# Router's logits in four groups of token tiles, behind the output projection of token tile 0

## What is computed

```python
def phi(x):                                   # 8 heads, 64 wide, 128 features
    proj = einsum('bhsd,df->bhsf', x, w_phi)
    proj = proj - max(abs(proj), axis=-1)
    return concatenate([exp(proj), exp(-proj)])
num, den = phi(q) @ (phi(k).T @ v), phi(q) @ sum(phi(k))
x = num / (den + 1e-6)                        # linear attention, then 512 wide

gate = sigmoid(causal 5-tap convolution of x, per channel)
x = (gate * (x @ w_val)) @ w_out              # gated block

logits = x @ w_gate                           # 8 experts, top 1
local  = sigmoid(x @ w_local)                 # >= 0.5: keep the expert of the token before
out[s] = softmax(logits[s])[e] * (relu(x[s] @ w1[e]) @ w2[e])
```

## Time and profile before

| | us |
|---|---|
| median of 3 runs (lowest to highest) | 531.75 (531.22 to 534.05) |
| the profiled execution | 531.9 |
| its span | 530.2 |

### The profile page before, as it was taken

The page is one execution under the profiler, slowest core; times in us unless marked ns, Lnnn a source line. Parts: engine busy times, 40 slices in busy tenths (PEclk is TensorE's granted clock), DMA queues, the critical chain, the costliest instruction groups (busy, mean ns, idle before and its releaser), DMA issues. The chain is left out here.

```text
span 530.2 us, 13320 instructions
## 1 busy us (share of the span) xinstructions
PE 510.3 (96%) x5374; PEld 431.7 (81%) x5374; DVE 301.5 (57%) x492; ACT 261.8 (49%) x450; POOL 220.5 (42%) x224
## 2 busy tenths in 40 slices
PE   6999999999999999999999999999999999999993
PEld 5898999988989999678887787888887777888872
DVE  4686878878986554287505657422375578522231
ACT  2555676666786331564625556322555557422330
POOL 3069999999999950436620001100111011100001
PEclk9999999999999999999999999999999999999998
DMA  8466464654510000006669399111382977111101
GB/s 298 133 201 208 139 227 157 203 189 139 165 70 1 0 1 1 1 1 205 253 239 337 106 351 339 61 40 40 102 295 50 348 278 265 41 40 42 53 25 43
DMA packets 31351, 75.34 MB, mean 142 GB/s; under 512 B 4159, under 2 KB 4415, under 8 KB 31296
## 3 DMA queue, kind: packets, MB, share of 16 engines
q1 hardware_dynamic: 25600, 60.37, 33.8%
q0 software_dynamic: 3104, 9.46, 4.6%
q10 hardware_dynamic: 2592, 4.74, 3.1%
HBM read 57.46 MB, written 17.55 MB: 141 GB/s over the span
## 5 line engine op out<-in xcount | busy, mean ns | idle before, releaser
L568 POOL TENSOR_TENSOR gate<-gate,tap 128x576 f32<-128x576 f32 x64 | 93.1, 1455 | 5.3
L612 POOL DMA_INDIRECT out_rows<-o_sb,meta_cur x18 | 18.6, 1033 | 151.5 <-DVE o_sb L1448 151.5
L1435 DVE TENSOR_TENSOR h_t<-pair_ps,h_t 128x512 fp32r<-128x512 f32 x36 | 24.9, 691 | 88.5 <-ACT h_t L1175 88.5
L662 PE MATMUL turn<-wts,h_t 128*128 128x512 f32 x144 | 60.0, 417 | 1.4 <-issue 1.4
L662 PE MATMUL num_ps<-wts,y_t 128*128 128x512 f32 x144 | 59.5, 413 | 0.1
L663 PE MATMUL turn<-wts,h_t 128*128 128x512 f32 x144 | 56.9, 395 | 0.0
L663 PE MATMUL num_ps<-wts,y_t 128*128 128x512 f32 x144 | 56.9, 395 | 0.0
L664 PE MATMUL turn<-wts,h_t 128*128 128x512 f32 x144 | 56.9, 395 | 0.0
L664 PE MATMUL num_ps<-wts,y_t 128*128 128x512 f32 x144 | 56.9, 395 | 0.0
L1209 DVE TENSOR_REDUCE absmax<-pair_ps 128x8 f32<-128x1024 f32 x31 | 38.0, 1225 | 29.8 <-PE pair_ps L671 29.8
L1167 ACT ACTIVATE h_sb<-num_ps 128x512 f32<-128x512 f32 x36 | 21.5, 598 | 65.6 <-PE num_ps L664 65.6
(11 more groups left out here) (210 smaller groups left out, 1117.6 us busy)
## 6 DMA issues: line engine op xcount, KB each, us to landing
ring<-in_w SPq DMA_DIRECT2D x36, 512.0 KB, 6.9
stage<-in_w SPq DMA_DIRECT2D x28, 512.0 KB
kq_t<-in_kq SPq DMA_DIRECT2D x15, 576.0 KB, 6.4
sorted_rows<-padrow SPq DMA_DIRECT2D x9, 771.0 KB, 5.7
v_sb<-in_v_aug SPq DMA_DIRECT2D x16, 325.0 KB, 3.2
ysl<-sorted_rows ACTq DMA_DIRECT2D x18, 257.0 KB
wout_t<-in_w_out_t SPq DMA_DIRECT2D x1, 1024.0 KB, 7.9
wval_sb<-in_w_val SPq DMA_DIRECT2D x1, 1024.0 KB, 9.5
```

The lines of the kernel that those rows point to most:

```text
L568: nc.gpsimd.tensor_tensor(g, g, tap[:, t % 2, :], ALU.add).then_inc(conv_step, 1)
L662: nc.tensor.matmul(dst, x[0], w[0], start=first, stop=False)
```

## The change

The constants: four groups of token tiles instead of three, the first two of 5 tiles and the others of 4. So the first piece is 4 groups of 512 columns, the second 2 groups of 128. The logits are computed behind tile 0 of the output projection instead of before it, and are transposed behind the second channel group of tile 1 instead of behind tile 0: five transposes, of 128 rows (the last of 64) instead of six of 96. The routing steps begin one tile later. ScalarE rounds tiles 0 and 1 as soon as the first batch is gated (in its queue that is behind the work of the last batch), into the buffers that do not overlap the weights of the value projection: `rounded(t)` turns the four buffers by two. The copy of the transposed logits becomes five instructions. GpSimd takes the low parts of 11 tiles instead of 9 and does its `iota` behind the fourth of them, no longer behind the last value tile. VectorE takes 7, the early weight chunks move by two tiles, and the eighth is subtracted behind the last low part.

```diff
-    LG = 3
-    LGS = TOK // LG
-    LGT = TT // LG
+    LG = P // LGW
+    LG_TILES = [TT // LG + (j < TT % LG) for j in range(LG)]
+    LG_AT = [sum(LG_TILES[:j]) for j in range(LG)]
+    LGT = LG_TILES[0]
+    LGS = LGT * P
+    WIDE = TT % LG
+    LG_HALF = 3
...
-        lg_pieces = [(kv_ps, slice(0, 512)), (num_ps[:, 0, :], slice(512, LGS))]
+        lg_pieces = [(kv_ps, slice(0, 512), LG), (num_ps[:, 0, :], slice(512, LGS), WIDE)]
...
-        POOL_LO = TT // 2
+        POOL_LO = TT // 2 + 2
         early_at = [i if i < STAGES else POOL_LO + 2 + i - STAGES for i in range(EARLY)]
...
+        EARLY_OUT = 2
+        def rounded(t):
+            return gs[(t + GS - EARLY_OUT) % GS]
...
-            pool.wait_ge(val_ok, B * 2 * CT)
-            nc.gpsimd.iota(ytok[:, :, C:C + 1].bitcast(I32), pattern=[[P, TT], [0, 1]], base=0,
-                           channel_multiplier=1).then_inc(conv_step, 1)
-            pool.wait_ge(conv_step, done + 1)
             for t in range(POOL_LO):
                 pool.wait_ge(g_hi, t + 1)
                 whole, (hi, lo) = split_gated(t)
                 nc.gpsimd.tensor_tensor(lo, whole, hi.bitcast(F32), ALU.subtract).then_inc(g_lo[0], 1)
+                if t == GS - 1:
+                    nc.gpsimd.iota(ytok[:, :, C:C + 1].bitcast(I32), pattern=[[P, TT], [0, 1]], base=0,
+                                   channel_multiplier=1).then_inc(conv_step, 1)
+            pool.wait_ge(conv_step, done + 1)
...
-            pe.wait_ge(gated_ok, B * 2 * CT)
-            for bank, at in lg_pieces:
-                w = at.stop - at.start
-                for c in range(CT):
-                    for j in range(LG):
-                        ins = nc.tensor.matmul(bank[j * LGW:(j + 1) * LGW, 0:w], wog[:, c, :],
-                                               gate[:, c, j * LGS + at.start:j * LGS + at.stop],
-                                               start=(c == 0), stop=(c == CT - 1))
-                ins.then_inc(lg_ok, 1)
+            def logits():
+                pe.wait_ge(gated_ok, B * 2 * CT)
+                for bank, at, groups in lg_pieces:
+                    w = at.stop - at.start
+                    for c in range(CT):
+                        for j in range(groups):
+                            ins = nc.tensor.matmul(bank[j * LGW:(j + 1) * LGW, 0:w], wog[:, c, :],
+                                                   gate[:, c, LG_AT[j] * P + at.start:LG_AT[j] * P + at.stop],
+                                                   start=(c == 0), stop=(c == CT - 1))
+                    ins.then_inc(lg_ok, 1)
...
                     if c == CT - 1:
                         ins.then_inc(y_ok, 1)
-                    if c % 2 == 1 and 0 <= 2 * t + c // 2 - 4 < len(routing):
-                        route(*routing[2 * t + c // 2 - 4])
+                    if t == 1 and c == 1:
+                        turn_logits()
+                    if c % 2 == 1 and 0 <= 2 * t + c // 2 - 6 < len(routing):
+                        route(*routing[2 * t + c // 2 - 6])
                 if t == 0:
-                    turn_logits()
+                    logits()
...
+            act.wait_ge(gated_ok, 2 * CT)
+            for t in range(EARLY_OUT):
+                round_gated(t)
             act.wait_ge(gated_ok, B * 2 * CT)
-            for t in range(GS):
+            for t in range(EARLY_OUT, GS):
                 round_gated(t)
-            for i, (bank, at) in enumerate(lg_pieces):
-                act.wait_ge(lg_ok, i + 1)
-                nc.scalar.copy(lg_rows[:, at], bank[0:LG * LGW, 0:at.stop - at.start]).then_inc(lg_read, 1)
             for t in range(TT):
                 act.wait_ge(y_ok, t + 1)
                 nc.scalar.copy(ytok[:, t, 0:C], turn_ps[t % 2][:]).then_inc(y_read, 1)
                 if t == 0:
+                    for i, (bank, at, groups) in enumerate(lg_pieces):
+                        act.wait_ge(lg_ok, i + 1)
+                        nc.scalar.copy(lg_rows[0:groups * LGW, at], bank[0:groups * LGW, 0:at.stop - at.start]).then_inc(lg_read, 1)
                     act.wait_ge(lg_ok, len(lg_pieces) + 1)
...
+                    read_logits()
...
                 if t - POOL_LO < EARLY:
                     rest_of_weights(t - POOL_LO)
+            for i in range(TT - POOL_LO, EARLY):
+                rest_of_weights(i)
```

More of the change, by code:

```diff
@@ L81, in attention_moe_kernel @@
     FEWT = E * FEW // P
-    LGT = TT // LG
-    assert LG * LGT == TT and LGT % 2 == 0 and E + 1 <= LGW
+    LG = P // LGW
[5 more added lines that the diff above has]
+    LG_HALF = 3
+    assert 0 < WIDE and LG_HALF < LGT - 1 and 512 < LGS < 1024 and (LGT - 1) * P == 512 and E + 1 <= LGW
     assert PAIRS == B * CT and FEAT == P and FULL * P + HALF == S and FULL * P == 512
@@ L398, in split_gated @@
         def split_gated(t):
-            return gate[:, :, t * P:(t + 1) * P], [gs[t % GS][:, i] for i in range(2)]
+            return gate[:, :, t * P:(t + 1) * P], [rounded(t)[:, i] for i in range(2)]
+        EARLY_OUT = 2
+        def rounded(t):
+            return gs[(t + GS - EARLY_OUT) % GS]
         block = ctx.enter_context(nc.Block())
@@ L820, in turn_logits @@
                 for i in range(LGT):
-                    ins = nc.tensor.transpose(lgt_ps[i // (LGT // 2)][:, i % (LGT // 2) * LG * LGW:(i % (LGT // 2) + 1) * LG * LGW],
-                                              lg_rows[:, i * P:(i + 1) * P], ident[0:LG * LGW, 0:LG * LGW])
+                    rows = P if i + 1 < LGT else WIDE * LGW
+                    at = i % LG_HALF * P
+                    ins = nc.tensor.transpose(lgt_ps[i // LG_HALF][:, at:at + rows],
+                                              lg_rows[0:rows, i * P:(i + 1) * P], ident[0:rows, 0:rows])
                 ins.then_inc(lg_ok, 1)
@@ L853, in _ @@
                 for c in range(CT):
-                    ins = product(turn_ps[t % 2][:], [gs[t % GS][:, j, c, :] for j in range(2)],
+                    ins = product(turn_ps[t % 2][:], [rounded(t)[:, j, c, :] for j in range(2)],
                                   [w[:, c, :] for w in (wout_hi, wout_lo)], c == 0, c == CT - 1)
@@ L1113, in round_gated, with read_logits @@
                 nc.scalar.copy(hi, whole).then_inc(g_hi, 1)
+            def read_logits():
+                for a in range(2):
+                    for j in range(0, LG, WIDE):
+                        n = min((a + 1) * LG_HALF, LG_TILES[j]) - a * LG_HALF
+                        rows = lg[:, LG_AT[j]:LG_AT[j] + WIDE * LG_TILES[j], :].rearrange("p (j i) e -> p j i e", j=WIDE)
+                        if a * LG_HALF + n < LGT:
+                            src = lgt_ps[a][:, 0:n * P].rearrange("p (i j x) -> p j i x", i=n, j=LG)[:, j:j + WIDE, :, 0:E + 1]
+                            nc.scalar.copy(rows[:, :, a * LG_HALF:a * LG_HALF + n, :], src).then_inc(lg_read, 1)
+                        else:
+                            for i in range(n):
+                                src = lgt_ps[a][:, i * P + j * LGW:i * P + (j + WIDE) * LGW].rearrange("p (j x) -> p j x", j=WIDE)
+                                nc.scalar.copy(rows[:, :, a * LG_HALF + i, :], src[:, :, 0:E + 1]).then_inc(lg_read, 1)
+            act.wait_ge(gated_ok, 2 * CT)
+            for t in range(EARLY_OUT):
+                round_gated(t)
             act.wait_ge(gated_ok, B * 2 * CT)
-            for t in range(GS):
+            for t in range(EARLY_OUT, GS):
                 round_gated(t)
-            for i, (bank, at) in enumerate(lg_pieces):
-                act.wait_ge(lg_ok, i + 1)
-                nc.scalar.copy(lg_rows[:, at], bank[0:LG * LGW, 0:at.stop - at.start]).then_inc(lg_read, 1)
             for t in range(TT):
@@ L1308, in _ @@
             V = nc.vector
-            dve.wait_ge(lg_read, len(lg_pieces) + 2)
+            dve.wait_ge(lg_read, len(lg_pieces) + 5)
             lgr = lg[:, :, 0:E]
```

5 lines of the change are left out of this document (removed).

## The result

The changed kernel takes 533.49 us in the median (530.27 to 536.15, 22 runs), the kernel before 531.75 in the same series (530.7 to 534.08, 22 runs). The ratio is 1.0027, with a 95% interval of 1.0015 to 1.0039: 0.3% slower, within the 0.5% that counts as no difference here, but on the other side of the forecast. 530.5 was forecast, with 529.3 to 532.2 as its range. The profiled execution took 534.0 us with a span of 532.3, at a granted clock of 0.996.

What follows compares the result with a forecast made beforehand. TensorE's own queue, busy for 96% of the span, was taken as the bound almost everywhere. The terms summed as 531.9 - 0.70 - 0.84 + 0.08 + 0.05 = 530.5 us, with 529.3 to 532.2 for 8 in 10.

Steps and rivals of the forecast that it cites:

- part 1: Between value projection and logits on TensorE: output projection tile 0 moves up and fills the gap, gain 0.70 us.
- part 2: Router's logits on TensorE: four column groups instead of three take 4.45 us instead of 5.29, gain 0.84 us.
- rival (d): Logits on TensorE: the fourth column group is paid in full, +1.1 us, total 531.6 us; chance 0.05.
- Rival (e): Start of output projection: tile 0 does not start at once, the 0.70 us stay, total 531.2 us; chance 0.06.
- Rival (f): Routing steps find everything ready and the logits take 4.0 us, total about 529.5 us; chance 0.07.
- part 3: Small terms around the logits: one more change of matmul shape +0.08 us, larger transposes +0.05, ACT's later copies 0.
- Tile 2's copy on ScalarE: Output projection: the copy ends near 227.1, tile 4 is due near 228; cover 1 us, cost 0.
- part 4: Routing steps on TensorE, moved from tile 2 to tile 3: no change in cost, bounds -0.5 and +0.5 us.
- The skill's rule: VectorE and GpSimd lock shared SBUF ports per instruction: two added subtractions would hold the routing chain 2.6 us, against 1.1 taken.
- What is late next: Routing chain, scatters and first expert's load: scatters 2.6 us later, but rows land near 267.2, before TensorE needs them at 267.9.
- (b): Expert stage's first rows: GpSimd's sequencer does not run ahead, TensorE waits 1.0 us, total 531.5 us; chance 0.18.
- (c): Expert stage's first rows: scatters go at the slow 1.74 us pace, TensorE waits 4.2 us, total 534.7 us; chance 0.06.

## Why the prediction was wrong, point by point

**The gap** (part 1): right, tile 0 starts 0.12 us behind the value product, and ScalarE's early casts lie in its idle time. **The logits** (part 2): right, 4.43 us against 4.45 forecast. The rival (d), a fourth group paid in full, is refuted by this and by the run with four groups alone. **Rival (e)**, the gap staying: refuted by the row of tile 0. **Rival (f)**, all routing steps ready, is refuted by the gap at the scan (its sum starts from 530.4 where the forecast is 530.5).

**The transposes** (part 3) are the first mis-sized term: +0.28 us, not +0.05. I scaled by the volume of data, and wrongly: by the shapes in the traces (96x96; 128x128 and 64x64) it is 26% more and not 16, which would be 0.12 us. The same 0.73 us is there in both kernels with four groups in the old place. Tile 2's copy on ScalarE was no wait, as said.

**The routing steps** (part 4) failed. "I change nothing there; bounds -0.5 (no waits at all) and +0.5": it is +1.03. The mechanism stood in the text, with its price of about 1 us, and I placed tile 5's subtraction rightly in VectorE's wait. But I followed the subtractions only as a delay of the positions and didn't put tile 6's, 1.95 us behind tile 5's, against the one scan for which TensorE itself waits. The run that moves it shows the gap gone.

**The skill's rule.** From VectorE's first copy of the routing to the first scatter it took 243.09 - 225.28 = 17.81 us, before 240.79 - 225.15 = 15.64: 2.2 us more where I took 1.1. The rule of "SBUF — State Buffer" in the Trainium skill, section "SBUF: two separate sides", gave 2.6 for both added subtractions held in full. The run with nine subtractions parts the sum: its stretch is 15.76, so 2.05 us belong to the two added ones, nearer to the rule than to my 1.1. The first scatter hit the forecast's 243.4 (243.09) only because this execution was 1.44 us ahead at the anchor: counted from there it is 1.1 us later than forecast.

**What is late next.** This is the step that decided. I forecast a TensorE 1.4 us earlier and scatters 2.6 us later, 4.0 us of lag, and the trace has 3.9. That match is luck: from the anchor TensorE is 0.2 us earlier at tile 12 and the scatters are 3.7 later (33.58 against 29.84), since the scan and the dearer subtractions were missed. I asked of the lag only whether the scatters would be in DRAM when the first rows are loaded. They were: the last low part decided the issue, as I said. The step that failed is the next one: "the rest of the program follows it rigidly as long as nothing else is late there" took for granted that TensorE's own signals are on time. They were up to 3.8 us late, TensorE stood, and through ScalarE's casts the last low part came 2.1 us later than before.

**Rivals (b) and (c)** have the right place, the wait for the first rows (1.6 us), and the wrong mechanism: neither GpSimd's mark nor its pace but the low part was late (SyncE's last wait ahead of the load is for VectorE's gs). Their prices would have added to a gain that was no longer there. Nothing in the trace of before could show a late signal, since there the scatters don't lag; what could be seen is that the change widens by 4 us a distance that held at its old width.

The two losses meet a gain of 1.58 us less small terms. With the scan it is nearly used up (0.20 us left at tile 12), and the late signals turn it into a loss that varies between executions: 0.7 to 3.5 us by the account from the anchor.

## What to carry to other kernels

A gap on the bounding engine is best filled with the part of the waiting work that is already ready: putting the wait in front of the one step that needs it kept the order of everything else and brought 0.7 us at tile 12 (43.64 from the anchor, where four groups alone have 44.30), while moving the whole block behind a tile cost more than it gave (533.13 with nine subtractions, where four groups in the old place have 530.81). When a change shifts two chains against each other, list each long instruction of one engine against every instruction of the other for which the bounding engine waits, not only against the chain's end. And treat a growing distance between a producer and its scatters as a risk of its own, shown so far in this kernel alone, to be tried with a single added wait, as here, before the change is built.

## What the hardware showed

- Four column groups cost what three cost: 512 fp32 columns in four groups took 3.46 us for the first piece (212.49 to 215.95), 0.43 for each of its eight steps, as three groups did.
- TensorE's semaphore updates came 0.8 to 3.8 us behind the end of the matmul that makes them, for tiles 13 to 17, when indirect DMAs of 128 rows of 2056 bytes lagged 1.8 us or more further behind; with 8 bytes a row they came within 0.02 us.
- A scan of 18x128 takes 0.39 us alone and 1.42 beside GpSimd's subtraction with three SBUF operands, a 128x18 tensor_scalar 1.09 beside one and 0.18 alone.
